# Two products of 64 rows instead of one of 128 rows with zeros, in the attention scores of an attention and mixture-of-experts kernel

## What is computed

```python
# B, H, S, D = 2, 8, 768, 64; block, window = 32, 16; nb = 24
k_sum = k.reshape(B, H, nb, block, D).max(axis=3)
v_sum = v.reshape(B, H, nb, block, D).mean(axis=3)
scores_l = scale * q @ k.T            # kept where |i - j| < 16
scores_s = scale * q @ k_sum.T + log(block)
a = softmax(concatenate([scores_l, scores_s], axis=-1))
x = a @ concatenate([v, v_sum])
# x goes to 1536 rows of 512; moe: each token to one of 8 experts
# (w_gate 512x8, w1 512x1024, relu, w2 1024x512), 192 tokens each;
# then h = x @ w_in; solu = h * softmax(h); layer norm; @ w_out
```

## Time and profile before

| | us |
|---|---|
| median of 3 runs | 519.24 |
| the profiled execution | 519.47 |
| its span, first to last instruction | 517.7 |
| attention, first scores to last router products | 6.5 to 110.4 |

### The profile page before, as it was taken

How to read it: one execution, slowest core, us unless ns; L and a number is a source line. 1 busy time by engine, 2 the same in 40 slices (tenths; PEclk the granted TensorE clock), 3 DMA queues, 4 the chain that set the end, 5 groups by cost and what they waited for, 6 DMA issues and landing times.

```text
span 517.7 us, 8533 instructions
## 1 busy us (share of the span) xinstructions
PE 455.9 (88%) x2810; PEld 401.2 (77%) x2810; DVE 340.9 (66%) x1169; ACT 162.0 (31%) x422; POOL 144.4 (28%) x201
## 2 busy tenths in 40 slices
PE   4999999960179996899999999999998999999992
PEld 2778788850169886887998987899897789899771
DVE  4677777669879879789769788976976530400340
ACT  2767777730021031123213113411411231231330
POOL 3697787910130220121122113122102323010001
PEclk9999999995569999799999999999999999999997
DMA  9867675110080450432045045015404509000001
GB/s 256 328 224 248 229 221 151 32 31 0 1 322 33 157 200 0 149 116 113 20 164 194 20 158 191 30 29 190 163 18 165 211 24 352 2 20 1 0 22 41
DMA packets 25604, 62.45 MB, mean 121 GB/s; under 512 B 6625, under 2 KB 14177, under 8 KB 21473
## 3 DMA queue, kind: packets, MB, share of 16 engines
q0 software_dynamic: 6592, 39.85, 21.1%
q1 hardware_dynamic: 18112, 21.13, 12.7%
q10 hardware_dynamic: 864, 1.02, 0.7%
HBM read 55.70 MB, written 6.29 MB: 120 GB/s over the span
## 4 chain that ended last, share of the span: by engine, by line
PE 71%; DVE 19%; issue 3%; ACT 3%; DMA 1%; SPq 1%; POOL 0%; ACTq 0%; DVEq 0%; POOLq 0%
PE psum L986 12%; PE psum L969 12%; DVE key_wide L1275 8%; PE psum L811 5%; PE psum L1031 5%; PE psum L1038 4%; PE psum L1032 4%; PE psum L1006 4%; PE psum L1007 4%; PE psum L1011 4%; PE psum L836 3%; PE psum L820 3%; PE psum L863 2%; PE psum L833 2%; PE psum L916 2%
## 5 line engine op out<-in xcount | busy, mean ns | idle before, releaser
L986 PE MATMUL psum<-xs,w_sb 128*128 128x192 f32 x512 | 89.5, 334 | 0.0
L1275 DVE TENSOR_SCALAR_CACHE_REDUCE key_wide<-keys,thr 128x1536 bf16<-128x1536 f32 x49 | 88.7, 1810 | 1.1
L969 PE MATMUL psum<-shared,w_sb 128*128 128x192 f32 x512 | 86.3, 330 | 1.2 <-ACT shared L711 1.2
L969 PEld LDWEIGHTS psum<-shared,w_sb 128*128 128x128 f32 x512 | 85.1, 193 | 2.0 <-issue 1.5
L986 PEld LDWEIGHTS psum<-xs,w_sb 128*128 128x128 f32 x512 | 85.5, 195 | 0.0
L599 POOL DMA_INDIRECT w_sb<-w,widx x32 | 31.1, 971 | 129.1 <-DVE widx L1350 87.3
L811 PE MATMUL psum<-w_sb,shared 128*128 128x376 f32 x96 | 43.5, 539 | 6.8 <-DMA w_sb<-k_win 6.8
L623 POOL TENSOR_TENSOR gain<-spread,cst 128x1 f32<-128x1 f32 x12 | 6.8, 568 | 150.0 <-DVE spread L1411 150.0
L1158 DVE CUSTOM_DVE_ANT_0 keys<-psum,w_sb 128x184 f32<-128x184 f32 x96 | 29.7, 348 | 25.5 <-PE psum L811 18.1
L1378 DVE TENSOR_TENSOR yT_lo<-psum,yT_hi 128x384 fp32r<-128x384 f32 x16 | 8.9, 555 | 53.6 <-ACT yT_hi L711 53.4
L674 ACT ACTIVATE keys<-keys,nmax 128x184 f32<-128x184 f32 x96 | 42.0, 441 | 4.7 <-DVE nmax L1158 4.7
(11 more groups left out here) (147 smaller groups left out, 829.9 us busy)
## 6 DMA issues: line engine op xcount, KB each, us to landing
shared<-kT SPq DMA_DIRECT2D x8, 384.0 KB, 5.3
shared<-vT SPq DMA_DIRECT2D x8, 384.0 KB, 6.1
shared<-v_main SPq DMA_DIRECT2D x8, 384.0 KB, 3.1
x_rows<-xs SPq DMA_DIRECT2D x8, 384.0 KB, 4.3
shared<-qT SPq DMA_DIRECT2D x7, 384.0 KB, 4.7
w_sb<-w_in SPq DMA_DIRECT2D x4, 512.0 KB, 6.0
w_sb<-w_out SPq DMA_DIRECT2D x8, 256.0 KB, 4.4
shared<-v_tail SPq DMA_DIRECT2D x16, 48.0 KB, 3.2
```

The costliest lines, as they stand in the source:

```text
L969: mm = pe.matmul(turn[u % 2][:, i * CAP:(i + 1) * CAP], w1_sb[:, par, first:first + P], xT[:, c, :], start=(c == 0), stop=(c == KC - 1))
L986: mm = pe.matmul(turn[u % 2][:, (d % 2) * CAP:(d % 2 + 1) * CAP], w2_sb[:, par, first:first + P], hT[:, c, :], start=(c == 0), stop=(c == ...
L1275: link(dve.tensor_scalar(hits, keys[:, :], cand, -float(CAP), ALU.is_ge, ALU.add, accum_out=count[:, :]))
```

## The change

Each head gets a product of its own: 64 rows of `q_sb` as the stationary operand, 184 columns of `kwin`, which now has no zeros and is 184 columns a tile. The products of units rotate through three banks, 0, 1 and 7: head `h` of unit `u` is in bank number `(2u + h) % 3` of these. The banks of unit `u` are then those of head 1 of unit `u-2` and head 0 of unit `u-1`, and so `scores(u)` waits for the masking of head 0 of the unit just before. Bank 7 is taken from the values: both halves of `pvo` now lie in bank 6, and `values(u)` waits for the division of unit `u-1`. The four memsets are gone.

```diff
-SUM0, SUM1 = KEYS, HEAD1
-TAIL1 = HEAD1 + NBLK
+SUM0, SUM1 = KEYS, 0
...
-        kwin = [w[:, 1, 0:QT * SCOLS].rearrange("p (t c) -> p t c", t=QT) for w in (w1_sb, w2_sb)]
+        kwin = [w[:, 1, 0:QT * COLS].rearrange("p (t c) -> p t c", t=QT) for w in (w1_sb, w2_sb)]
...
-        score = bank[0:2]
+        score = [bank[0], bank[1], bank[7]]
...
-        pvo = [pv[:, 0:P], small[:, 0:P]]
+        pvo = [pv[:, 0:P], pv[:, P:2 * P]]
...
-                sp.dma_start(kwin[0][D:P, tiles, TAIL1:SCOLS], windows[D:P, tiles]).then_inc(landed, 16)
+                sp.dma_start(kwin[0][D:P, tiles, NBLK:COLS], windows[D:P, tiles]).then_inc(landed, 16)
...
-            pool.memset(kwin[1][0:D, :, COLS:SCOLS], 0.0).then_inc(k_zeroed, 1)
-            pool.wait_ge(k_zeroed, 1)
-            pool.memset(kwin[1][D:P, :, 0:HEAD1], 0.0).then_inc(k_zeroed, 1)
-            pool.wait_ge(k_zeroed, 2)
...
-                if u >= 2:
-                    pe.wait_ge(masked, 2 * (u - 1) + 2 * LOOP_UN * it)
-
-                pe.matmul(score[s][:, 0:SCOLS], q_sb[:, b, t * P:(t + 1) * P], kwin[b][:, t, :], start=True,
-                          stop=True).then_inc(scores_ready, 1)
+                if u >= 1:
+                    pe.wait_ge(masked, 2 * u - 1 + 2 * LOOP_UN * it)
+                for h in range(2):
+                    rows = slice(h * D, h * D + D)
+                    mm = pe.matmul(score[(2 * u + h) % 3][:, 0:COLS], q_sb[rows, b, t * P:(t + 1) * P], kwin[b][rows, t, :],
+                                   start=True, stop=True)
+                mm.then_inc(scores_ready, 1)
...
-                if u >= 2:
-                    pe.wait_ge(x_ready, u - 1 + LOOP_UN * it)
+                if u >= 1:
+                    pe.wait_ge(x_ready, u + LOOP_UN * it)
...
-            pe.wait_ge(zeroed, 3)
+            pe.wait_ge(zeroed, 1)
...
-                    dve.tensor_tensor_reduce(neg[:, s, hh, :], score[s][:, HEAD1 * hh:HEAD1 * hh + COLS],
+                    dve.tensor_tensor_reduce(neg[:, s, hh, :], score[(2 * u + hh) % 3][:, 0:COLS],
...
-            dve.memset(kwin[0][0:D, :, COLS:SCOLS], 0.0).then_inc(zeroed, 1)
-            dve.memset(kwin[0][D:P, :, 0:HEAD1], 0.0).then_inc(zeroed, 1)
```

More of the change, by code:

```diff
@@ L303, in build @@
         v_zeroed = sem("v_zeroed")
-        k_zeroed = sem("k_zeroed")
         kmax_ready = sem("kmax_ready")
@@ L489, in key_windows @@
                     pool.wait_ge(scores_ready, QT * (g - 1))
-                for h, col in enumerate((0, TAIL1)):
+                for h, col in enumerate((0, NBLK)):
                     rows = slice(h * D, h * D + D)
@@ L883, in step @@
                     turn_gated(gate_block(u), it)
-            pe.wait_ge(zeroed, 3)
+            pe.wait_ge(zeroed, 1)
             for u in range(LOOP_U0):
                 step(u)
-            pe.wait_ge(k_zeroed, 2)
             pe.wait_ge(in_gate, 32)
```

## The result

The changed kernel takes 525.57 us in the median of 20 runs (521.49 to 528.62), the kernel before 520.93 on the same chip (20 runs, 518.9 to 523.35): ratio **1.0096, 95% interval 1.0072 to 1.0119**. It is slower by 0.7 to 1.2%. The forecast of 520.0 us was too low: against the 0.8 us that its sum added stand 4.6 between the medians.

What follows compares the result with a forecast made beforehand. TensorE's queue was taken to bound attention. -1 us (product), +1.3 (`key_max` stalls) and +0.5 (last values) gave +0.8: 519.47 to 520.2 us profiled, 520.0 in the median; range 517 to 530.

Steps and rivals of the forecast that it cites:

- the partial overlap: Rival for the scores: only head 0's second record runs beside head 1's first, +0.154 us a unit, 526.5 us; chance 0.29.
- full overlap with two switches: Main case: both heads' scores run wholly side by side, each unit paying two row-count switches; 516 to 523 us, chance 0.51.
- The product: Scores in attention: overlap saves 0.31 us a unit, two switches take 0.29; -0.02 a unit, -1 us for 48.
- no overlap: Rival for the scores: heads run one behind the other and still pay both switches, 0.29 us a unit, 533.5 us; chance 0.10.
- no emptying: Last rival: row-count switches don't empty the array, attention's ordinary step falls by 0.31 us to 1.32, 511 us; chance 0.09.
- The rule of strict order: Skill rule read as making head 1's first scores record wait for head 0's second; rejected from column-tile rows, full overlap taken.
- The mode switch: On TensorE, each change between 128 and 64 rows empties the array for 0.10 us, then leaves a load uncovered.
- The masks: Scores waiting for head 0's mask of the unit before: 1.29 us from load to load, under a step's 1.6, costs nothing.
- The wait for the division: Values waiting for the previous unit's division: slack 0.4 us, except behind some `key_max` (1.3 us) and at the end (0.5).
- 3 x 0.42 = 1.3 us: Values stalled 0.42 us each behind `key_max` at units 14, 26 and 38, where no router work stands between.
- +0.5 us: Last values of attention: unit 47's start at 106.61, but unit 46's division ends at 107.05; all on the path.
- The start: First scores: the second ones now wait for a mask that begins 0.6 us earlier, so end no later; cost 0.

Runs made afterwards that it cites:

- run 9: Changed kernel with both heads' products on head 0's rows, so one row tile and no overlap: 571.29 us in the median of two runs.
- run 3: Changed kernel with each head's scores in a bank of its own (0 and 1), values in two banks with the old wait: 520.45 us, ratio 1.0008.
- run 6: Changed kernel with `key_max` and the value mean issued behind the step's reciprocal and division: 521.77 us, ratio 1.0019.
- run 7: Changed kernel with the edits of run 5 and run 6 together: 520.03 us, ratio 1.0002.
- run 5: Changed kernel with unit 47's values sent to bank 0, not waiting for the division of unit 46: 522.61 us, ratio 1.0048.
- run 1: Kernel before, with only the values' halves sharing bank 6 and waiting for the previous unit's division: 524.84 us, ratio 1.0069.
- run 2: Changed kernel's banks and waits, but each head's product takes 128 rows, with zeros in the other head's: 525.54 us, ratio 1.0081.
- run 4: Changed kernel with 54 small bf16 products of ones on TensorE before the first scores: 524.68 us, ratio 1.0078.
- run 10: Changed kernel with twelve bf16 products of ones in each of the first five steps: 523.28 us, ratio 1.0049.
- run 11: Run 3 with 50 products of ones ahead of the scores and fillers in the first five steps: 519.59 us, ratio 0.9983.
- run 12: Kernel before with 50 products of ones ahead of the scores and fillers in the first five steps: 520.15 us, ratio 1.0000.
- run 8: Run 3 with `value_sum` issued one tile earlier (tile 3 instead of 4): 522.68 us, ratio 1.0019.

## Why the forecast was too low

**The range: held by luck.** Its upper part, up to 530, stood there for the partial overlap (526.5), and that is excluded below. The case that came true, full overlap with two switches, had a range of its own, 516 to 523, and 525.57 lies outside it. (Three of the rivals' totals are 0.1 to 0.2 us off as sums, which changes nothing.)

**The product: right.** Full overlap, and two switches that eat it. The plain step is 1.61 us as worked out; without overlap it is 1.91 (run 9). With the waits gone attention is 1.2 us shorter (runs 3, 6, 7), 1 forecast. The rivals of partial overlap (step 1.76), no overlap (1.91) and no emptying (1.32) are each excluded by the step.

**The rule of strict order: misread.** The Trainium skill's section "What overlaps and what doesn't" (TensorE: Matmul & The Clock Gate, Part 3) has matmuls start and end in program order. The prediction took that for single records, and for records the trace of the changed kernel disagrees: the first two of a step's four records start 7 ns apart and the other two 0.25 us later, also 7 ns apart, where on one tile (run 9) no two start less than 0.15 us apart. Taken for whole products the rule agrees with this trace: the last record of the second product starts, and by the profile ends, 7 ns behind that of the first. Between run 9 and the changed kernel the same four records differ by 0.31 us.

**The mode switch: right.** The rule that a change of tiling mode drains the engine (the Trainium skill, TensorEngine Tiling (Array Packing), Key Properties) is borne out: 0.26 us between the last load of 128 rows and the first of 64, and 0.51 from there to the next load of 128 rows, of which the two overlapped records are 0.31.

**The masks: right in attention.** In no step of steady attention does TensorE wait for line 1153 in a way that lengthens it: the waits between 16 and 104 us show none, and the plain step is the sum of its own work.

**The wait for the division: the step that failed, in two places.** The sum had "3 x 0.42 = 1.3 us" and "+0.5 us".
- For `key_max` it held: 3 x 0.45 = 1.35. But "a `value_sum` is waited for already (...) I add nothing" left out the value mean of the step behind it, which the same prediction did count in its last rival. Its 0.46 us stand between a mask and its division. The steps of units 18, 30 and 42 lose 0.33, 0.28 and 0.11, together 0.7. The 0.11 is the mean alone; what makes the mask late in front of the other two isn't shown. It isn't the sum, which ended at 43.98 us in the first of them, 1.13 before that mask: there VectorE stands idle for 0.31 us with no releaser on record, in the first step of a round of the hardware loop. Run 6 gives all of it back: 82.54 becomes 80.52.
- In the tail the wait was 0.55 us, but the stretch grew by 2.1: the clock fell inside it. Run 5, without this wait, has the tail at 8.50 us and full clock. In all seven profiles in which the last values wait (the changed kernel, runs 1, 2, 4, 6, 9 and 10) the clock falls 1.7 to 4.8 us before the last router product. In the seven in which they don't, it falls 7.9 to 9.2 us behind that product in four (the kernel before, runs 3, 5 and 11) and close to it in three: 0.9 behind (run 7), 0.3 behind (run 12) and 0.5 before (run 8). So the early fall went with the wait every time, but taking the wait out doesn't by itself put the fall off by much, and the 1.6 us beyond the wait itself are the clock's cost in one profiled execution.

Together this is 2.0 + 2.1 = 4.1 us where 1.8 stood, and with the waits out the ratio goes from 1.0096 to 1.0002 (run 7). With the product's own 1.2 us won (run 3) and the 1.7 us of the start below, -1.2 + 2.0 + 2.1 + 1.7 = 4.6 us, the difference of the medians. The terms come from single profiled executions, so that they add up this closely is in part chance.

**The start: "0" was too little.** I compared the ends of the second scores and not TensorE's load. The products on half the rows leave idle time for the masks, and the clock rose at 21.2 us instead of 16.3. Not in every execution: it rose between 14.8 and 17.1 in three profiles of kernels with products of 64 rows and no warming or filling (runs 3, 6, 7), at 21.2 to 49.0 in four (the changed kernel, runs 5, 8 and 9), and at 15.4 to 16.3 in the three of 128-row kernels. That thinner work is what delays it is argued, not shown: TensorE is busy for 6.82 of the 8 us from 8 to 16 in run 8, where the clock rose at 27.9, and for 6.15 in run 6, where it rose at 15.6. Filling the steps gives 1.0049 for 1.0096, a difference of 2.4 us. It says about what the start costs in the mean and settles it no closer, since the fillers may win more than the change lost. In run 3, whose attention is 1.2 us shorter than before, the median is no shorter, and its single executions hint why: seven lie at 517.7 to 520.5 us, the profiled one with its early clock the fastest of them, and five at 521.9 to 524.4. Run 8 has five at 517.7 to 519.3 and seven at 521.6 to 524.7, the profiled one with its late clock among these. With the first steps filled (run 11) all twelve lie at 517.8 to 520.6. That the upper groups are those with the late clock would need their profiles.

**What stays open.** Behind attention the profiled execution is 3.5 us longer. The program is the same there, and the two profiled executions differ by 3.6 us more than the medians, so most of this need not be the change's. From the last router product to the last matmul are 400.6 to 401.0 us in three profiles (the changed kernel, runs 6 and 10), the only ones in which the clock has a spell of 3.4 us at 1.2 GHz some 70 us behind that product (185.1 us in the changed kernel); the other eleven have 397.3 to 399.6, four of them kernels whose last values wait. What brings that spell no run told.

## What to carry to other kernels

When two buffers move into one bank, the writer waits for the reader of the other half: list everything that the reader's engine does ahead of that read, in every step and after every late instruction, and issue the read first. A short wait in a stretch where TensorE is thin can cost more than itself if the clock falls there: here 2.1 us for 0.55 in the profiled execution. Splitting a product with zeros into row tiles saves half its stream, but each visit to another tile size pays for emptying the array twice: here 0.29 us of 0.31. By these figures it would pay where many such products follow each other, which no run here tried.

## What the runs showed of the hardware

- Two fp32 products on different 64-row halves run wholly beside each other, each as two records, and the second product's first record passes the first product's second one: four records in 0.58 us, 0.89 on the same half.
- Changing between 128 and 64 rows cost what the turning of tokens had shown, for another operation and another shape: a plain step of 1.61 us, as worked out from them.
- TensorE's granted clock, once at 2.4 GHz, was lost at 11.5 us behind 5.4 us with 1.96 of work (run 4), and a wait of 0.55 us in the tail went with a fall some 9 us earlier (110.0 for 118.7). Without that wait the clock still fell within 1 us of the last router product in three of seven profiles.
